# Router of a fused attention and two-expert-layer kernel worked per chunk of two tiles, with a shorter index step, output zeros written mid-run and the first expert's rows and weights taken ahead

## The reference, cut to what matters

```python
x = _attn_ref(q, k, v, n_sink=4, window=128)      # (2, 8, 768, 64) -> (1536, 512)
h = x @ w_in                                      # 512 -> 2048
y = (np.maximum(h, 0) + alpha * np.minimum(h, 0)) @ w_out
logits = y @ w_gate                               # 8 experts
expert_idx = np.argmax(logits, axis=1)
gate_w = softmax(logits)[np.arange(N), expert_idx]
for i in range(N):                                # in order of tokens
    e = expert_idx[i]
    if counts[e] < capacity:                      # capacity 384: three tiles of 128
        disp[e, counts[e]] = y[i]; pos[i] = counts[e]; counts[e] += 1; keep[i] = True
z = np.einsum('ecf,efd->ecd', np.maximum(np.einsum('ecd,edf->ecf', disp, w1), 0), w2)
out[i] = gate_w[i] * z[expert_idx[i], pos[i]] if keep[i] else 0
```

## Time and profile before

| | |
|---|---|
| median of 3 runs | 667.24 us (666.74 to 668.3) |
| the profiled execution's own time | 664.13 us |
| its span in the profile | 662.4 us |
| what lies around the span | 1.73 us |
| instructions | 11777 |
| PE busy | 599.6 us (91%) |
| DVE busy | 372.3 us (56%) |
| ACT busy | 286.9 us (43%) |
| POOL busy | 158.7 us (24%) |
| mean granted clock of PE | 0.964 |
| HBM over the span | 106 GB/s |

### The profile page before, as it was taken

How to read it: one execution, slowest core, us unless ns; L and a number is a source line. 1 busy time by engine, 2 the same in 40 slices (tenths; PEclk the granted TensorE clock), 3 DMA queues, 4 the chain that set the end, 5 groups by cost and what they waited for, 6 DMA issues and landing times.

```text
span 662.4 us, 11777 instructions
## 1 busy us (share of the span) xinstructions
PE 599.6 (91%) x3875; PEld 506.2 (76%) x3875; DVE 372.3 (56%) x1133; ACT 286.9 (43%) x681; POOL 158.7 (24%) x213
## 2 busy tenths in 40 slices
PE   7779899999999999999999999929999789859983
PEld 6668788888888888888888898728777667647772
DVE  4657767666567656655664465373943644654410
ACT  4665554433343334333432221233854755565520
POOL 5653222222222222222221000032121321330112
PEclk9899999999999999999999999958999999979997
DMA  7533340201020102010000400195865675966100
GB/s 208 145 81 96 120 120 18 65 17 35 17 64 17 33 17 65 17 33 17 33 17 1 159 1 1 57 288 180 286 235 178 212 231 185 293 210 205 58 33 18
DMA packets 73394, 67.37 MB, mean 102 GB/s; under 512 B 43012, under 2 KB 49172, under 8 KB 73328
## 3 DMA queue, kind: packets, MB, share of 16 engines
q1 hardware_dynamic: 69488, 57.76, 28.1%
q0 software_dynamic: 3840, 8.77, 4.7%
HBM read 57.75 MB, written 12.58 MB: 106 GB/s over the span
## 4 chain that ended last, share of the span: by engine, by line
PE 79%; DVE 6%; issue 6%; ACT 5%; DMA 1%; POOL 1%; ACTq 0%; DVEq 0%; POOLq 0%
PE bank L810 21%; PE bank L812 20%; PE bank L811 20%; PE bank L800 8%; PE bank L847 4%; PE bank L873 4%; ACT fw L639 2%; PE bank L941 1%; DVE wl L1085 1%; ACT wh L618 1%; DMA fw<-y_scratch,v_or_route 1%; DVE rw L1103 1%; PE bank L887 1%; ACT rw L624 0%; DVE fw L1257 0%
## 5 line engine op out<-in xcount | busy, mean ns | idle before, releaser
L810 PE MATMUL bank<-wh,rw 128*128 128x512 f32 x416 | 169.7, 408 | 10.7 <-issue 6.2
L812 PE MATMUL bank<-wh,rw 128*128 128x512 f32 x416 | 163.9, 394 | 0.0
L811 PE MATMUL bank<-wl,rw 128*128 128x512 f32 x416 | 163.8, 394 | 0.0
L1085 DVE TENSOR_TENSOR wl<-fw,wh 128x512 fp32r<-128x512 f32 x160 | 100.3, 686 | 36.7 <-ACT wh L618 34.8
L810 PE MATMUL bank<-rw,wh 128*128 128x256 f32 x384 | 113.2, 295 | 0.0
L812 PE MATMUL bank<-rw,wl 128*128 128x256 f32 x384 | 108.7, 283 | 0.0
L811 PE MATMUL bank<-rw,wh 128*128 128x256 f32 x384 | 108.6, 283 | 0.0
L720 ACT CAST rw<-fw 128x256 fp32r<-128x256 f32 x96 | 39.0, 406 | 150.8 <-DVE fw L1262 150.7
L810 PEld LDWEIGHTS bank<-wh,rw 128*128 128x128 f32 x416 | 79.1, 190 | 28.1 <-issue 13.1
L812 PEld LDWEIGHTS bank<-wh,rw 128*128 128x128 f32 x416 | 78.8, 189 | 17.6
L618 ACT CAST wh<-fw 128x512 fp32r<-128x512 f32 x160 | 87.9, 619 | 5.6 <-DMA fw<-in_moe_w_dram 2.5
(11 more groups left out here) (140 smaller groups left out, 670.6 us busy)
## 6 DMA issues: line engine op xcount, KB each, us to landing
fw<-in_moe_w_dram SPq DMA_DIRECT2D x128, 256.0 KB
fw<-in_moe_w_in_dram SPq DMA_DIRECT2D x16, 256.0 KB, 3.4
fw<-in_moe_w_out_dram SPq DMA_DIRECT2D x16, 256.0 KB, 2.9
o_sb<-in_q_dram SPq DMA_DIRECT2D x12, 256.0 KB, 3.4
o_sb<-in_k_dram SPq DMA_DIRECT2D x12, 256.0 KB, 4.1
y_scratch<-fw SPq DMA_DIRECT2D x12, 256.0 KB, 2.1
out_dram<-v_or_route SPq DMA_DIRECT2D x12, 256.0 KB, 3.0
v_raw<-in_v_dram SPq DMA_DIRECT2D x11, 256.0 KB, 3.1
```

The costliest lines, as they stand in the source:

```text
L810: pe.matmul(dst, ah, bh, start=start, stop=False, skip_group_check=True)
L811: pe.matmul(dst, ah, bl, start=False, stop=False, skip_group_check=True)
L812: return pe.matmul(dst, al, bh, start=False, stop=stop, skip_group_check=True)
L1085: dve.tensor_tensor(wl[:, hf, col:col + PIECE], staged, f32(wh[:, hf, col:col + PIECE]), ALU.subtract).then_inc(weights_low_split, 1)
```

## The change

The router works on a chunk: one pass of DVE for two tiles, with buffers that are two tiles wide. `y_T` of the two tiles stands in steps 0 and 2, `logits` of both in step 3, `ranks` of both in step 4 and `slots` in step 6; `choose` still stands between the two activation operations and the low part, `rank` and `tables` behind it. The table holds the token number itself, plus one, in place of tile and row, so that it has 2 and not 3 parts; the gather's indices come from it in one operation and the scatter's in two more. POOL starts gathering at the first of the three.

Behind the last step, ACT copies one of the two tiles of y and DVE the other, and the same for their transposes. Three of the first expert's pieces (`FIRST`) are split ahead of that, in the last step. PE gets transposes of the identity, into a bank that nobody reads, between the router's matmuls and five behind each of the 8 register loads (`keep_busy`, L802). On ACT and DVE the first tile's split stands ahead of the register loads. The first expert's hidden layer is made in two halves of columns, and the transpose of the second tile of rows stands between them. The zeros are written one block a step in the third chunk.

```diff
+        last_y_evacuated = sem("last_y_evacuated")
+        last_yT_evacuated = sem("last_yT_evacuated")
         NCONST = 16
-        RS = 17
-        NIX = 6
+        RS = 26
+        CHOSEN, RANKED, COUNTED, PLACED = 8, 10, 18, 24
+        NIX = 3
+        FIRST = 3
...
+                if c == 2 and i < NT:
+                    if i == 0:
+                        sp.wait_ge(zero_rows_made, 1)
+                    sp.dma_start(out[i * P:(i + 1) * P, :].rearrange("p (a n) -> p a n", a=KC),
+                                 zero_sb[:, :].unsqueeze(1).to_broadcast([P, KC, P])).then_inc(output_zeroed, 16)
...
-            sp.wait_ge(zero_rows_made, 1)
-            for t in range(NT):
-                sp.dma_start(out[t * P:(t + 1) * P, :].rearrange("p (a n) -> p a n", a=KC),
-                             zero_sb[:, :].unsqueeze(1).to_broadcast([P, KC, P])).then_inc(output_zeroed, 16)
...
-            pool.wait_ge(index_steps, NIX)
+            pool.wait_ge(index_steps, 1)
...
             pool.wait_ge(output_zeroed, 16 * NT)
+            pool.wait_ge(index_steps, NIX)
...
-            def __init__(self, eng):
+            def __init__(self, eng, between=None):
                 self.eng = eng
                 eng.wait_ge(counts_in_sbuf, 1)
-                self.count = [eng.value_load(counts[0:1, e:e + 1], min_val=0, max_val=N) for e in range(E)]
+                self.count = []
+                for e in range(E):
+                    self.count.append(eng.value_load(counts[0:1, e:e + 1], min_val=0, max_val=N))
+                    if between is not None:
+                        between()
 
...
-            def router_exp(t):
-                b = Routed(t)
-                act.wait_ge(*steps_of(t, 1))
-                act.activation(b.el, b.lg, ACT.Exp, bias=b.rs[:, 0:1], scale=1.0,
-                               accum_out=b.rs[:, 1:2]).then_inc(router_exp_done, 1)
+            def router_exp(c):
+                act.wait_ge(router_steps, RS * c + 4)
+                for tt in range(TPC):
+                    act.activation(el[:, :], lg[:, tt, :], ACT.Exp, bias=rs[:, 0, tt:tt + 1], scale=1.0,
+                                   accum_out=rs[:, 1, tt:tt + 1]).then_inc(router_exp_done, 1)
...
-                for tt in range(TPC):
+                for tt in range(TPC - (c == NC - 1)):
...
+                if c == NC - 1 and i == NF - 1:
+                    some(FIRST, 0)
...
+            some(KC * FP2 - FIRST, 0)
+            x_high(0)
             busy = Busy(act)
-            x_high(0)
             busy.run(x_high, 1, slot_x_high_split)
...
-            def logits(t, n):
-                pe.wait_ge(yT_evacuated, t + 1)
+            def logits(c, n):
                 pe.wait_ge(scores_masked, min(2 * (n // 2) + 2, NH))
-                b = Routed(t)
-                for kk in range(KC):
-                    r = pe.matmul(b.logits, b.yT[:, kk, :], wg[:, kk, :], start=(kk == 0), stop=(kk == KC - 1))
+                for tt in range(TPC):
+                    pe.wait_ge(*yT_copied(TPC * c + tt))
+                    for kk in range(KC):
+                        r = pe.matmul(LOGITS[:, tt * E:(tt + 1) * E], yT[:, tt, kk, :], wg[:, kk, :],
+                                      start=(tt == 0 and kk == 0), stop=(tt == TPC - 1 and kk == KC - 1), skip_group_check=True)
                 r.then_inc(logits_done, 1)
...
+            def ranks(c):
+                pe.wait_ge(router_steps, RS * c + CHOSEN)
+                pe.matmul(RANKS, tri[:, :], oh[:, :, :].rearrange("p s e -> p (s e)"),
+                          start=True, stop=False, skip_group_check=True)
+                pe.matmul(RANKS, ones[:, :], ohsum[:, :].unsqueeze(1).to_broadcast([P, TPC, E]),
+                          start=False, stop=False, skip_group_check=True)
+                pe.matmul(RANKS[:, E:2 * E], ones[:, :], oh[:, 0, :],
+                          start=False, stop=True, skip_group_check=True).then_inc(ranks_done, 1)
+
+            def slots(c, n):
+                pe.wait_ge(router_steps, RS * c + PLACED)
                 pe.wait_ge(scores_masked, min(2 * (n // 2) + 2, NH))
...
+                for tt in range(TPC):
+                    r = pe.matmul(SLOTS, ohb[:, tt, :], ins[:, tt, :, :].rearrange("p a b -> p (a b)"),
+                                  start=tt == 0, stop=tt == TPC - 1)
+                r.then_inc(slots_done, 1)
...
-                if c >= 1 and i < 4 * TPC:
-                    ROUTE[i % 4](TPC * (c - 1) + i // 4, n)
+                if c >= 1 and i in (0, 2):
+                    y_T(TPC * (c - 1) + i // 2, n)
+                if c >= 1 and i == 3:
+                    logits(c - 1, n)
+                if c >= 1 and i == 4:
+                    ranks(c - 1)
+                if c >= 1 and i == 6:
+                    slots(c - 1, n)
...
-
+            pe.wait_ge(activation_done, NF * NC)
+            keep_busy(3)
+            for t in range(NT - TPC, NT):
+                y_T(t, NH)
+            logits(NC - 1, NH)
+            keep_busy(8)
+            ranks(NC - 1)
+            keep_busy(8)
+            pe.wait_ge(router_steps, RS * (NC - 1) + COUNTED)
             pe.matmul(P_BANK[:, 0:E], ones[:, :], ohsum[:, :], start=True, stop=True).then_inc(experts_counted, 1)
-            pe.wait_ge(counts_in_sbuf, 1)
-            busy = Busy(pe)
+            keep_busy(4)
+            slots(NC - 1, NH)
+            keep_busy(6)
+            busy = Busy(pe, lambda: keep_busy(5))
...
             slot_T(0)
+            keep_busy(10)
+            expert_in(0, (0,))
             busy.run(slot_T, 1, slot_x_transposed)
-            expert_in(0)
+            expert_in(0, (1,))
             busy.run(slot_T, 2, slot_x_transposed)
...
+                step(dve.tensor_copy(lg[:, :, :].rearrange("p s e -> p (s e)"), LOGITS))
+                upto(1)
+                for tt in range(TPC):
+                    step(dve.max(top[:, tt, :], lg[:, tt, :]))
+                upto(3)
+                step(dve.tensor_scalar(negmax, top[:, :, 0], -1.0, None, ALU.mult))
+                for tt in range(TPC):
+                    step(dve.max_index(topi[:, tt, :], top[:, tt, :], lg[:, tt, :]))
                 upto(6)
+                step(dve.tensor_copy(idx, topi[:, :, 0]))
+                upto(7)
+                step(dve.tensor_tensor(oh[:, :, :], iota[:, 0:E].unsqueeze(1).to_broadcast([P, TPC, E]),
+                                       idx.unsqueeze(2).to_broadcast([P, TPC, E]), ALU.is_equal))
...
+                step(dve.tensor_scalar(sumexp, sumexp, 1e-9, None, ALU.add))
+                upto(19)
+                step(dve.reciprocal(id_gate[:, :, 1], sumexp))
+                for tt in range(TPC):
+                    step(dve.tensor_scalar(ohb[:, tt, :], iota[:, :], off[:, tt:tt + 1], None, ALU.is_equal))
+                upto(20)
+                for tt in range(TPC):
+                    step(dve.scalar_tensor_tensor(out=ins[:, tt, :, :], in0=iota[:, 0:NA].unsqueeze(1).to_broadcast([P, 2, NA]),
+                                                  scalar=place[:, tt:tt + 1],
+                                                  in1=id_gate[:, tt, :].unsqueeze(2).to_broadcast([P, 2, NA]),
+                                                  op0=ALU.is_equal, op1=ALU.mult))
...
+                dve.wait_ge(router_steps, RS * c + PLACED)
+                step(dve.tensor_scalar(id_gate[:, :, 0], id_gate[:, :, 0], float(TPC * P), None, ALU.add))
+                dve.wait_ge(slots_done, c + 1)
+                step(dve.tensor_tensor(inv[:, :, :], inv[:, :, :],
+                                       SLOTS.rearrange("p (a b) -> p a b", a=2), ALU.add))
...
-                if c >= 1 and i < 4 * TPC and i % 4:
-                    ROUTE[i % 4](TPC * (c - 1) + i // 4)
+                if c >= 1 and i == 3:
+                    choose(c - 1)
                 if 0 <= m < NF * NC:
                     dve.wait_ge(activation_high_split, m + 1)
                     dve.tensor_tensor(g_hl[m % 2][:, 1, :], g_full[:, m % 2, :], f32(g_hl[m % 2][:, 0, :]),
                                       ALU.subtract).then_inc(activation_low_split, 1)
+                if c >= 1 and i == 4:
+                    rank(c - 1)
+                if c >= 1 and i == 6:
+                    tables(c - 1)
                 for p in range(split_by(n - 1), split_by(n)):
                     weights_low(p)
 
...
+            some(FIRST, 0)
+            dve.wait_ge(y_stored, 16 * TPC * (NC - 1))
+            dve.wait_ge(y_transposed, TPC * (NC - 1))
+            dve.wait_ge(y_done, NF * NC)
+            dve.tensor_copy(y_sb[:, TPC - 1, :], Y_BANK[TPC - 1][:, :]).then_inc(last_y_evacuated, 1)
+            dve.wait_ge(logits_done, NC - 1)
+            dve.wait_ge(y_transposed, NT)
+            dve.tensor_copy(yT[:, TPC - 1, :, :], yT_bank(NT - 1)[:, :].rearrange("p (c n) -> p c n", c=KC)).then_inc(last_yT_evacuated, 1)
+            choose(NC - 1)
+            rank(NC - 1)
```

(8 more changed lines are left out.)

255 lines of the change are left out of this document (93 added, 162 removed).

## The result

| | before | changed |
|---|---|---|
| median of 14 runs each, side by side | 666.48 us (664.21 to 669.93) | 662.52 us (658.86 to 664.87) |
| ratio, 95% interval | | 0.9936 (0.9915 to 0.9957) |
| the profiled execution's own time | 664.13 us | 661.42 us |
| its span | 662.4 us | 659.7 us |
| mean granted clock of PE | 0.964 | 0.978 |

The changed kernel is faster, by 4.0 us, and inside the range; 7.05 us were forecast. PE is busy for longer since it now works through fillers, and DVE is busy for 14.5 us less.

The account below looks back on a forecast made before the run. PE was taken as the bound, by its work and few idle places. Gains 2.0 + 4.6 + 0.9 - 0.45 = 7.05 us took the profiled 664.13 to 657.1; plus 3.11 for the median, 660.2 us, range 656.0 to 665.0.

Parts of the forecast that it names:

- y to first matmul: Last `y_sum` to the first expert's first matmul: earlier index, shorter gather and hidden loads bring it 4.6 us earlier.
- Routing of earlier chunks: Router steps of the chunks: 1.0 us gained in the last, 0.25 in each of four ahead; 2.0 us, bounds 1.3 and 6.
- The rival by which it does nothing in mid-run: Zeros and chunk router move nothing as PE is the bound: 0 to 0.3 us, 662.0; chance counted within forecast's 0.58.
- Zeros in mid-run: Twelve zero writes, one per third-chunk step behind loads of q, k, v: cost nothing; at most 1.4 us twice.
- The gather: POOL's first gather, start to rows: 4.5 us, between 3.5 and 5.66; rows at 441.9 us.
- The index: Last two tiles' router: first gather index at 436.5 us, 2.2 earlier; POOL starts at 437.4.
- the clock falls all the same: Rival, router to first expert: PE at 1.2 GHz, first matmul only 0.7 us earlier, slow pace stays; 665.4 us, chance 0.12.
- Register loads and fillers: PE's eight loads, five fillers behind each, overlap: 6.4 us, bounds 5.4 and 9.6; PE free at 442.4, 0.5 behind rows.
- the rival of a series: PE's register loads and fillers run one after the other at full clock: gain 1.8 instead of 4.6 us; 663.0, chance 0.13.
- the slower case: Fillers in series with PE's loads at half clock: 13.7 us of rounds, 2.6 us slower overall; 669.8, chance 0.04.
- Pace of the first expert: First expert's matmuls 0.23 us apart in place of 0.43: 0.9 us saved, less 0.45 for the second transposes.
- Given back in the experts: Rival, first expert: 0.7 us of cover goes and second-half weights are late, 2 to 3 us return; 662.7, chance 0.10.

Follow-up runs that it names:

- second profile: Unaltered reruns for another trace: the changed kernel, 662.74 us, ratio 0.9957; the kernel before, 665.71 us, ratio 0.9991.
- zeros late: Changed kernel with the twelve blocks of zeros written behind the last `store_y` again, ahead of the weights: 664.34 us, ratio 0.9974.
- holding the pieces: Changed kernel, but SP loads weight pieces 11 and on only when the second gather has landed: 660.73 us, ratio 0.9923.
- without fillers: Changed kernel with all of PE's fillers between the last `y_sum` and the first expert removed: 663.38 us, ratio 0.9968.
- DVE after: Changed kernel with pieces held back, DVE's five remaining differences moved behind the first tile's low part: 660.00 us, ratio 0.9891.
- warm gather: Changed kernel with pieces held back, plus an unread POOL gather of 128 rows of `w2` in the last chunk: 660.68 us, ratio 0.9897.
- the last version: As the three together, with three fillers per register load, not five, and three ahead, not six: 656.91 us, ratio 0.9864; again 656.27 us, 0.9863.
- the three together: Changed kernel with held pieces, the early unread gather and DVE's differences behind the first tile's low part: 659.95 us, ratio 0.9911.

## Why the prediction was right, and where not

The forecast's terms against what was measured. The first matmul is taken by the timeline, which has it 0.35 us earlier than the chain in the kernel before, so that its 4.6 has a measured 1.9 to 2.3 beside it:

| term | forecast | measured | from |
|---|---|---|---|
| router, last chunk | 1.0 | 1.1 | 27.51 less 26.39 us for eight steps |
| router, four chunks ahead | 1.0 | 0.9 | 323.1 less 322.2 us, from DVE's activation at 52.65 (now 50.97) to that at 375.71 (373.17), each with a stretch at half clock near 81 us |
| y to first matmul | 4.6 | 1.9 | 22.09 less 20.18 |
| pace, less the second transposes | 0.45 | 0.8 | fifth expert output behind the first matmul, 71.44 less 70.68 |
| sum | 7.05 | 4.7 | median: 4.0 |

The 1.9 us have three parts. POOL starts 1.85 us earlier behind y (13.01 less 11.16; 1.1 to 2.2 us by the other pairs of profiles), the way from the rows to the matmul is 1.36 us shorter (3.42 less 2.06), and the gather takes 1.3 us more (0.8 between the second profiles of the two).

**Routing of earlier chunks** was right in both halves, 2.0 us. This is the steadiest number of all: counted from the 16th activation behind the one at 52.65 on, up to the same end, it is 258.54 to 258.56 us in the three traces of the kernel before and 257.61 to 257.68 in the eleven with the change. The rival by which it does nothing in mid-run would have given 662.0, close to the median, but by another way: the term that it strikes out is there in full.

**Zeros in mid-run** at nothing was right to half a microsecond: the run with zeros late lost 0.5 in the trace. The loads of q, k and v lost nothing: the 16 activations of the third chunk take 64.87 us with the zeros in it and 64.88 in the run with zeros late.

**The gather is the step that failed**: "Pieces 11 to 15 are still loaded just then, so I take 4.5, in the middle." It took 6.96 and 6.16 in the two profiles, outside the bounds of 3.5 and 5.66. The second and third profiles of the kernel before have 5.36 and 5.35, so that the row of 5.66 was no low one. The upper bound was the row of before, which I put down to "zeros and weights". That reading is what was wrong. The issues of the zeros were over by 436.5 there and the DMA engines empty at 439.0 to 439.6, before POOL began; what stood beside its rows was a queue of pieces and DVE's differences, and those stand beside the gather of the changed kernel too, as the stretches show. So nothing had left, and there was no reason to go below 5.66. The forecast also had no term for what else a first gather costs: it added POOL's own row to the landing of a store. The runs size it, from 6.1 us (second profile, by the chain): holding the pieces takes off 0.9, a warm POOL 2.0 more, and DVE's differences 0.2 with POOL cold and nothing with it warm; a gather that stands alone and isn't the first lands in 3.4. In the second profile of the kernel before one part was late as well: fifteen of the sixteen landed by 4.57 us and the last at 5.32. Why 6.2 to 7.0 and not the 5.3 to 5.7 of before is in part POOL's own first instruction, 1.72 for 1.41; the other 0.2 to 1.3 us stays open.

**The index** was to be 10.8 us behind y, and was 11.16 and 11.92. The router's legs ran partly at half clock, 428.9 to 432.3 in the first profile and 428.4 to 435.2 in the second, where the forecast wanted a clock of 1.00 throughout; of its signs of being wrong this is the one that came. It is the rival "the clock falls all the same", in a small part: 0.3 and 1.1 us later than forecast, where the rival put 0.8, and without the slow pace behind it. Over all traces with the change POOL starts 11.16 to 11.18 us behind y in the two in which these legs with their fillers were at half clock for 3.4 us and in the one without fillers, and 11.80 to 12.04 in the eight in which it was 6.8. For PE what it did before the fall was short work with waits between: by the chain, from 426.92 to 428.33 it waits for `choose`, with 8 fillers in it, while no DMA is waited for.
The Trainium skill (TensorE: Matmul & The Clock Gate, section on why this matters) has it that copying out of PSUM does not break the clock. Taken as the prediction took it, with the router's waits as such copies, nothing would have fallen here, and the trace does not bear that out: the fall at 428.9 comes behind waits for DVE alone. These waits are for more than a copy, so whether the sentence fails or doesn't apply no run here shows.

**Register loads and fillers** were right: PE's loads ran from 431.8 to 437.1 beside 46 fillers, 0.71 us apart (the forecast's 0.65 was a misreading: its rows, 4.8 us for seven distances, give 0.69), and PE was free 2.83 us before the rows, so the rival of a series falls, and with it the slower case, which needed rounds of 1.3 us. The rule on PE's queue in the Trainium skill that the prediction cited (same page, section on the array's architectural detail) is now borne out by a row on PE itself. Behind the rows the first matmul took 2.06 us (441.04 to 443.10), where 2.5 were forecast.

**Pace of the first expert** was right, and the run without fillers shows it by its reverse: 0.43 apart to 446.1, 1.7 us lost.

**Given back in the experts** did not show. PE's chain has no wait for the second tile, and in the run with DVE after, with the weights later yet, 0.3 us came. The two profiled executions do differ by 2.9 us behind the first matmul, 213.7 us before and 216.6 now, and by 1.7 the other way ahead of the activation at 52.65 (now 50.97), which is why they are 2.7 us apart and not 4.7. But the three traces of the kernel before have 213.7, 216.5 and 216.3 there, and the two of the changed kernel 216.6 and 215.6: the first profile of before was the short one. A microsecond or two given back could not be told from this.

For the place between y and the matmul the account closes. 17.83 us were forecast for it and 20.18 measured: 0.33 for the index and 2.46 for the gather, less 0.44 behind it, make 2.35 (in the second profile 1.09 + 1.66 - 0.44, 2.31 of 2.31). In absolute time the miss looks smaller than it is, 662.5 for 660.2, as the kernel before ran 0.8 us faster beside it than on record: that is luck.

**That it would be faster** rested on several terms of one sign with PE as the bound, and each of these held but one, so a sum that is half as large again as what was measured left the direction alone.

What stays open: why one of the sixteen parts of a first gather lands 1.0 to 1.9 us behind the others, with no piece beside it and with DVE quiet, when after a warm gather none does; what the pieces would still cost a warm gather, which was not tried; and what makes the last version 3.0 us faster than the three together, where its place explains 0.9. Which share of it is fewer falls of the clock in the experts was not tried.

## What to carry to other kernels

A transfer's duration taken from a trace holds for what stood beside it then, so where a wait is all that is left on the path, list what the change puts beside it (issues of another queue, another engine's operations, the first use of an engine) and take the old row for a bound only when those are gone. When a latency becomes the bound, hold back the transfers that nobody waits for, and make one cheap use of the issuing engine earlier: the early gather of 128 rows was worth 2.0 us of landing here, and holding the pieces 0.9. Compare two traces part by part, as a stretch of half clock ahead of the place can look like the gain of an edit (0.7 of the 1.0 us with DVE after). Fillers that keep a clock up must end before what they wait for arrives: 19 fewer of them gave 0.9 us once the rows came early, and before that they hid half of what the warm gather won.

## What the runs showed of the hardware that was not expected

- POOL's first indirect gather took 1.72 us with five of DVE's differences beside it (1.41 in the kernel before, with eight), 1.25 without, and 1.00 when it was not the first.
- The rows of a first gather were complete 5.24 us behind POOL's start with no piece beside them, as one of sixteen parts came about 1 us behind the others, and those of a gather that was not the first 3.28 us.
- Five pieces of weights beside a gather of 128 rows made it 0.9 to 1.7 us longer.
- The same wait of PE is followed by 3.4 us at half clock in one execution and by none in another (the stretches at 570.4 and 561.2 above), which is worth 1.3 us each time; executions of the changed kernel lie between 658.86 and 664.87 us.
- Eight register loads on PE ran beside 46 queued fillers at 0.71 us each (431.8 to 436.8), as fast as in the run without fillers, where they started from 431.8 to 436.6.
